# Turning the hidden rows of a routed feed-forward layer through DVE squares and HBM, one expert slot at a time

## What is computed

```python
def _moe2_ref(x, expert_emb, tau, w1, w2):
    ...
    expert_idx = np.argmax(logits, axis=1)
    ...
    for e in range(E):
        mask = expert_idx == e
        ...
        h = np.maximum(x[mask] @ w1[e], 0.0)
        out[mask] = gate_w[mask, None] * (h @ w2[e])
```

## Time and profile before

| | us |
|---|---|
| median of 3 runs (525.84 to 526.74) | 526.49 |
| the profiled execution, its own time | 526.66 |
| its span, first to last instruction | 524.9 |
| TensorE busy in it | 511.5 |
| DVE, ScalarE, GpSimd busy | 332.2, 213.2, 92.5 |

### The profile page before, as it was taken

One profiled execution on the slowest core, in us unless ns is written; L12 is line 12 of the kernel. 1 busy time (PEld: TensorE's weight loads), 2 busy tenths in 40 slices (PEclk: granted clock), 3 DMA queues, 4 the chain that ended last, 5 costly groups with the idle time before them and its releaser, 6 DMA issues.

```text
span 524.9 us, 11573 instructions
## 1 busy us (share of the span) xinstructions
PE 511.5 (97%) x3754; PEld 439.7 (84%) x3755; DVE 332.2 (63%) x712; ACT 213.2 (41%) x480; POOL 92.5 (18%) x223
## 2 busy tenths in 40 slices
PE   8799999999999999999999999999999999999994
PEld 7588888888888888888898999887788888888883
DVE  3679899687867665767554568767573473222662
ACT  5668654433443334333432445441531441111440
POOL 6412121002340000000000001002221211111221
PEclk9999999999999999999999999999999999999999
DMA  8899415586445335332412710102964155101000
GB/s 193 259 340 314 89 35 117 133 150 122 105 117 109 66 66 138 74 61 51 120 42 61 301 41 18 33 33 72 353 225 168 40 183 191 40 29 37 20 20 25
DMA packets 125899, 60.24 MB, mean 115 GB/s; under 512 B 95382, under 2 KB 113814, under 8 KB 125856
## 3 DMA queue, kind: packets, MB, share of 16 engines
q1 hardware_dynamic: 123456, 53.38, 37.4%
q0 software_dynamic: 2400, 6.30, 3.6%
HBM read 50.22 MB, written 11.01 MB: 117 GB/s over the span
## 4 chain that ended last, share of the span: by engine, by line
PE 94%; SPq 2%; DMA 1%; issue 1%; ACT 1%; DVE 0%; POOLq 0%; DVEq 0%; ACTq 0%
PE bank L1051 26%; PE bank L1095 9%; PE bank L1102 9%; PE bank L1108 8%; PE bank L1258 5%; PE bank L1304 5%; PE bank L1266 5%; PE bank L1312 5%; PE bank L1260 5%; PE bank L1306 5%; PE bank L1029 3%; PE bank L1296 2%; PE bank L999 2%; DMA v_raw<-in_v 1%; PE bank L1163 1%
## 5 line engine op out<-in xcount | busy, mean ns | idle before, releaser
L1459 ACT ACTIVATE el<-bank 128x512 f32<-128x512 f32 x48 | 28.6, 597 | 98.4 <-PE bank L1051 98.1
L1051 PE MATMUL bank<-x_hi,w_hi_parts 128*128 128x256 f32 x376 | 60.8, 284 | 0.0
L1051 PE MATMUL bank<-x_lo,w_hi_parts 128*128 128x256 f32 x376 | 60.1, 282 | 0.0
L1051 PE MATMUL bank<-x_hi,w_lo_parts 128*128 128x256 f32 x376 | 60.0, 282 | 0.0
L1051 PEld LDWEIGHTS bank<-x_hi,w_hi_parts 128*128 128x128 f32 x376 | 53.4, 188 | 3.7 <-issue 0.2
L1783 DVE TENSOR_SCALAR el<-el 128x512 f32<-128x512 f32 x48 | 20.6, 429 | 55.0 <-ACT el L1459 55.0
L1095 PE MATMUL bank<-w_hi_parts,g_hi 128*128 128x512 f32 x192 | 54.9, 407 | 0.0
L1102 PE MATMUL bank<-w_lo_parts,g_hi 128*128 128x512 f32 x192 | 52.7, 396 | 0.0
L1108 PE MATMUL bank<-w_hi_parts,g_lo 128*128 128x512 f32 x192 | 52.2, 393 | 0.0
L789 POOL COPY kb<-kT 128x96 f32<-128x96 f32 x96 | 26.2, 316 | 143.7 <-PE bank L999 123.3
L1051 PEld LDWEIGHTS bank<-x_lo,w_hi_parts 128*128 128x128 f32 x376 | 51.3, 188 | 0.0
(11 more groups left out here) (292 smaller groups left out, 871.6 us busy)
## 6 DMA issues: line engine op xcount, KB each, us to landing
raw<-in_moe_w SPq DMA_DIRECT2D x8, 2048.0 KB, 8.9
w_raw<-in_moe_w_in SPq DMA_DIRECT2D x8, 512.0 KB, 6.4
w_raw<-in_moe_w_out SPq DMA_DIRECT2D x8, 512.0 KB, 6.5
p_rows<-p_all SPq DMA_DIRECT2D x16, 256.0 KB, 2.4
p_squares<-p_rows SPq DMA_DIRECT2D x64, 64.0 KB, 2.4
v_raw<-in_v SPq DMA_DIRECT2D x8, 384.0 KB, 4.5
x_rows<-x SPq DMA_DIRECT2D x6, 512.0 KB, 3.2
x<-x_rows SPq DMA_DIRECT2D x20, 128.0 KB, 2.8
```

Of the source, the lines that this page charges most:

```text
L1051: mm = pe.matmul(o, r32(w[:, at:at + P]), r32(x[i % 2][:, c, :]), start=(part == "hh" and c == 0), stop=(part == "lh" and c == DC - 1))
L1459: act.activation(el[n % 2], bank[:, H_BANK[n % 2], :], ACT.Exp).then_inc(e_act, 1)
```

## The change

From slot 2 on `h_sb` is no longer made by ScalarE and transposed by TensorE. DVE transposes the 32x32 squares of the two banks into `h_sb` (`turn_h`, before the ReLU), ScalarE's queue stores `h_sb` to a tensor `h_rows` in HBM (`store_h`) and loads it back in four pieces, each for 32 partitions, into `h_squares` (`load_h`). ScalarE takes the ReLU and the high part from there (`h_high`), DVE the low part in four pieces (`h_low`). A partition then holds other rows of `w2` than before, so `w2` is loaded in four DMAs of 32 partitions (on SyncE's queue), and slots 0 and 1 write `h_sb` in a permuted order.

`down(s)` now follows `up(s + 2)`. Ups of slots 2, 3 and 4 come before the loop, slot 3's in banks 2 and 3 with its own buffers for the turned rows; the last two downs come after the loop. `w1` of a new run is split one pass earlier (in pass s for a start at s+3), and run 1 is entered at slot 4. Slot s's result is stored by DVE behind the `h_low` of slot s+1.

```diff
@@ TensorE
             def up(s):
...
-                pe.wait_ge(h1_ev, s + 1)
+                if isinstance(s, int) and s == FILL:
+                    pe.wait_ge(h1_ev, FILL + 1)
+                elif isinstance(s, int) and s == FILL + 2:
+                    pe.wait_ge(h_turned, 1)
+                elif not isinstance(s, int):
+                    pe.wait_ge(h_turned, s - FILL)
...
+                if isinstance(s, int):
+                    transpose_x(s + 1)
+                up_low(range(HALVES), base, s).then_inc(h1_mm, 1)
...
-            up(2)
-            transpose_x(3)
-            transpose_h(2)
-            up(3)
-            transpose_x(4)
-            down(2)
+            third_last = pe.value_load(tab[0:1, USED, 1:2], min_val=NT - 3, max_val=NSLOT - 3)
+            up(FILL)
+            up(FILL + 1)
+            up(FILL + 2)
+            down(FILL)
             with pe.Fori(FILL + 1, NSLOT) as s:
-                with pe.If(s < used):
-                    transpose_h(s)
-                    with pe.If(s + 1 < used):
-                        transpose_x(s + 2)
-                        up(s + 1)
+                with pe.If(s + 2 < used):
+                    transpose_x(s + 3)
+                    up(s + 2)
                     down(s)
+            down(third_last + 1)
+            down(third_last + 2)
@@ ScalarE
+            def store_h(s):
+                act.wait_ge(h_turned, s - 1)
+                if not isinstance(s, int) or s > FILL:
+                    act.wait_ge(ld_h, 16 * GROUPS * (s - FILL))
+                    carry_waits(act)
+                act.dma_start(h_rows, h_sb).then_inc(st_h, 16)
+            def load_h(s):
+                act.wait_ge(st_h, 16 * (s - 1))
+                if isinstance(s, int) and s == FILL:
+                    act.wait_ge(r_mm, NB)
+                else:
+                    act.wait_ge(hT_ev, 2 * s + 2)
+                    carry_waits(act)
+                for r in range(GROUPS):
+                    act.dma_start(h_squares[r * SQ:(r + 1) * SQ, :].rearrange("p (g d) -> p g d", g=GROUPS),
+                                  h_rows[:, r * FC2 * SQ:(r + 1) * FC2 * SQ].rearrange("(g p) d -> p g d", p=SQ)
+                                  ).then_inc(ld_h, 16)
+            def h_high(s):
+                act.wait_ge(h2_high, s)
+                act.wait_ge(ld_h, 16 * GROUPS * (s - 1))
+                for a in range(2):
+                    act.activation(r32(of_half(hT_hi, a)), h_by_chunk(a), ACT.Relu).then_inc(hT_hi_a, 1)
...
-            relu_halves(FILL)
+            store_h(FILL)
             there, run = starting_run(act, slice(3, 4))
             with act.If(there > 0):
                 high_w1(run())
+            load_h(FILL)
+            there, run = starting_run(act, slice(4, 5))
+            with act.If(there > 0):
+                high_w1(run())
+            store_h(FILL + 1)
...
             with act.Fori(FILL, NSLOT) as s:
...
+                with act.If(s + 2 < used):
+                    h_high(s)
+                    load_h(s + 1)
+                    high_of_next(s)
+                    there, run = starting_run(act, s + 3)
                     with act.If(there > 0):
                         high_w1(run())
...
+                    store_h(s + 2)
+            h_high(third_last + 1)
+            load_h(third_last + 2)
+            high_of_next(third_last + 1)
+            h_high(third_last + 2)
@@ VectorE
+            def turn_h(s):
+                dve.wait_ge(h1_mm, s + 1)
...
+                    dve.wait_ge(st_h, 16 * (s - FILL))
+                b = banks_of_hidden(s)[0]
+                dve.transpose(h_sb, bank[:, b:b + 2, :].rearrange("p a n -> p (a n)")).then_inc(h_turned, 1)
+            def h_low(s):
+                dve.wait_ge(h2_mm, s + 1)
+                dve.wait_ge(hT_hi_a, 2 * s + 2)
+                for r in range(GROUPS):
...
+                    ins = dve.scalar_tensor_tensor(out=r32(lo), in0=rows, scalar=0.0, in1=hi,
+                                                   op0=ALU.max, op1=ALU.subtract)
+                ins.then_inc(hT_ev, 2)
...
-            store_xsT(3)
             store_y(1, list_gate[:, 0, 1:2])
+            dve.wait_ge(meta_v, 2)
+            store_xsT(FILL + 1)
+            turn_h(FILL)
...
+            store_xsT(FILL + 2)
+            there, run = starting_run(dve, slice(4, 5))
+            with dve.If(there > 0):
+                low_w1(run())
+            turn_h(FILL + 1)
...
+            h_low(FILL)
+            turn_h(FILL + 2)
+            store_xsT(FILL + 3)
             later_splits(FILL)
...
             with dve.Fori(FILL + 1, NSLOT) as s:
...
+                with dve.If(s + 2 < used):
+                    h_low(s)
+                    gated_y(s - 1)
                     later_splits(s)
...
+                    turn_h(s + 2)
+                    store_xsT(s + 3)
+            h_low(third_last + 1)
+            gated_y(third_last)
+            low_of_next(third_last + 1)
+            h_low(third_last + 2)
+            gated_y(third_last + 1)
+            gated_y(third_last + 2)
```

More of the change, by code:

```diff
@@ L325, in build @@
          _, _, emb, emb_n,
-         h_sb, hT_hi, hT_lo, slot_vals, _, xs_even) = zone(
+         h_sb, hT_hi, hT_lo, slot_vals, _, xs_even, _, h_squares) = zone(
             "x",
@@ L410, in starting_run, with banks_of_hidden, homes_of_turned_rows, h_by_chunk @@
             return load(0), lambda: load(1)
+        xsT_of_three = tuple(c_free[:, a * DM:(a + 1) * DM].rearrange("p (c n) -> p c n", c=DC) for a in range(2))
+        def banks_of_hidden(s):
+            return HT if isinstance(s, int) and s == FILL + 1 else H1
+        def homes_of_turned_rows(s):
+            return xsT_of_three if isinstance(s, int) and s == FILL + 1 else (xsT_hi, xsT_lo)
+        def h_by_chunk(a):
+            return h_squares.rearrange("p (r c t) -> p c r t", r=GROUPS, c=FC2)[:, 4 * a:4 * a + 4, :, :]
+        def of_half(x, a):
+            return x[:, 4 * a:4 * a + 4, :].rearrange("p c (r t) -> p c r t", r=GROUPS)
         def bank_of_rows(s):
@@ L1305, in down_high @@
                           start=(f == 0), stop=False)
-                pe.matmul(bank[:, 4, :], r32(hT_hi[:, f, :]), r32(W_LO[:, bass.ds(at, DM)]),
-                          start=False, stop=False)
+                return pe.matmul(bank[:, 4, :], r32(hT_hi[:, f, :]), r32(W_LO[:, bass.ds(at, DM)]),
+                                 start=False, stop=False)
             def down_low(s, a, base):
@@ L1589, in relu, with relu_half @@
                 act.wait_ge(h1_mm, s + 1)
[L1590 to L1593, removed]
+                act.wait_ge(h1_t, 2 * s)
+                relu_half(0)
+                relu_half(1).then_inc(h1_ev, 1)
+            def relu_half(a):
+                rows = h_sb.rearrange("p (c q f) -> p q c f", c=FC2, q=GROUPS)[:, 2 * a:2 * a + 2, :, :]
+                return act.activation(rows, bank[:, a, :].rearrange("p (q c f) -> p q c f", q=2, c=FC2), ACT.Relu)
             def hT_high(s):
@@ L1619, in _ @@
             store_x2T(1, S_BANK[1])
[L1620 to L1628, removed]
+            act.wait_ge(h1_half, 1)
+            relu_half(0)
+            act.wait_ge(h1_mm, 1)
+            relu_half(1).then_inc(h1_ev, 1)
             hT_high(0)
@@ L2160, in later_splits @@
                     low_w2(run())
-                there, run = starting_run(dve, s + 2)
+            def later_splits(s):
+                low_of_next(s)
+                there, run = starting_run(dve, s + 3)
                 with dve.If(there > 0):
```

108 lines of the change are left out of this document (57 added, 51 removed).

## The result

The changed kernel takes 571.32 us (median; 569.71 to 573.12) against 526.16 for the kernel before beside it: a ratio of 1.086, interval 1.083 to 1.089. It is 45 us slower. The direction was forecast, the size was not: 543.5 was forecast, and 571.3 lies above the range of 529 to 556. The profiled execution has a span of 568.0, 43.1 over the one before.

The account below looks back on a forecast made before the run. TensorE, 97% busy, was taken as the bound: 526.66 us, less 11.0 for the turns and a wait gone, plus 27.8 of new waits (way in, passes with a split, way out), gives 543.5; range 529 to 556.

Parts of the forecast that it names:

- passes with a split: Row turns wait for xsT behind DVE's and ScalarE's chain: 5.0 in pass 3, 3.2 in 4, 1.6 in 6, 2.4 in 10.
- the way in: Ahead of and entering the loop: the first down waits 5.5 us for slot 2's hidden rows, then down(3) 0.5.
- the way out: Last two downs wait for DVE's stored result: down(12) 5.1 us, skipped passes included, down(13) another 4.5.
- The three durations taken for the turn and the two parts: On DVE and ScalarE: turn_h 1.4 us, h_low 1.6, h_high 2 x 0.6.
- the price of the trip: Hidden rows through HBM: a 512 KB store lands after 3.2 us, a 128 KB load after 2.8.
- the clock: Rival, 15%: TensorE's clock falls in three gaps of 5 us or more, costing 8.4 us; time 552.
- w2 in four DMAs: On SyncE's queue: three more issues, about 1.4 us, with nothing queued behind them for a whole pass; no cost.
- a pass without a split: In the loop: DVE's and ScalarE's work fits, so a pass takes 11.6 us, nothing beyond the matmuls.
- The second up covers it: Rival, 12%: with brief issues on ScalarE, split passes nearly close; way in and passes lose under 3 us; time 524.4.
- Rows come late in every pass: Rival, 8%: GpSimd's gather behind the scatter takes 12.3 us, not 10.9 of 11.6; nine passes lose 0.7 each; 550.

Follow-up runs that it names:

- run 1: Not a follow-up run: within the kernel, the slots from slot 4 on that share one set of new weights w1 and w2; no measured time of its own.
- small weights: The changed kernel, loading only a sixteenth of every row of the new weights (outputs of their slots wrong): 553.2 us, ratio 1.052 to the kernel before.
- order and small weights together: The best order without holding back run 1's w2, and only a sixteenth of every row of the new weights loaded (outputs wrong): 523.8 us, ratio 0.997.
- the best order: The changed kernel with run 1's w2 load held back, casts before load_h, last two passes inside the loop, result stored before h_low: 538.9 us, ratio 1.026.

## Why the prediction was wrong

**Direction and mechanism held.** The chain through DVE and ScalarE in passes with a split, the way in, and the way out were all found where the steps put them: five waits for xsT behind passes 3, 4, 6, 10 (and a short one ahead of pass 3), one for `hT_hi`, two for `y_sb`. The three durations taken for the turn and the two parts were 4 to 12% high.

**The step that failed is the price of the trip.** "Going through HBM is shown for x_rows: a store of 512 KB lands after 3.2, a load of 128 KB after 2.8" was taken for every pass, with crowding granted in the way in alone, and there by 0.7 us in the sum. But new weights are loaded as soon as a split has freed their place, and the next trip starts behind the same split. So the trip behind each of the first splits is crowded, and it hurts where the next pass has a split too: stores took 9.8, 8.0 and 9.0 for slots 2, 3 and 5. Against the steps: first down 11.5 for 5.5; ahead of pass 3 1.7, where the steps had 0.5 at down(3); pass 3 3.3 for 5.0; pass 4 6.7 for 3.2; pass 6 2.5 for 1.6 and pass 10 2.9 for 2.4, both with an uncrowded trip; way out 7.8 for 9.6. With small weights these waits are 19.6 and the time 18 us less, where the steps without their crowding had 27.1. That is the control: the places were right, the price of the trip was too low, and what passes 3 and 4 lose without crowding had been put too high (2.1 for 8.7), which hid a part of the miss.

**The second is the clock.** By the table it is the larger part of the miss. The forecast had +16.8 and the span +43.1. Of these 26.3 us, 8.5 are the waits that the steps name (36.3 for 27.8), 3.5 those for "issue" less the rest of the waits before, and 14.3 the slow matmuls and what was not taken apart. In the run with small weights the slow matmuls come to 12.7, and it ends 10 us above the forecast though the loads crowd nothing. The clock stood among the rivals at 8.4 us for three gaps. It is not a rival but a part of the forecast: slow matmuls stood behind eight of the waits, the ones of 1.66 to 11.5 us, 10.1 us of slower matmuls. In the trace before it was only seen to fall late in an idle of 6 us, and so I counted only gaps of 5 us and more, and gave the whole a chance of 15%. The price on the path is smaller than the sum (nothing at the first gap, about 1.4 us in the way out). The Trainium skill (TensorE: Matmul & The Clock Gate, HAM oscillation) describes bursts that start cold behind a long wait for DMA; the windows of 0.53 and 1.00 above agree.

**Third, two terms at nothing.** w2 in four DMAs was costed at 1.4 us of SyncE's time with nothing behind it; alone, with the permuted rows, it costs 5 us on the kernel before, where ScalarE is behind its landing. And a pass without a split was put at 11.6; with short waits for "issue" ahead of its up (0.53 in pass 9), whose cause was not looked for, passes 8 and 9 took 11.8 and 12.5. Such waits are 4.0 us in all, 1.2 of it ahead of the loop.

**The rivals.** "The second up covers it" fell: four issues hold ScalarE's queue 1.8 us, as SyncE's were held. The rule on issuing engines (the Trainium skill, DMA: Bandwidth & Descriptors, Issuing engines are not separate DMA queues) calls that small relative to the DMA; here it is 1.8 beside a landing of 2.9, and the traces disagree with "small". The same section says that DMAs of all issuing engines run on the same 16 DMA engines and interleave; the stores of ScalarE's queue that took 8.0 to 9.8 us beside a load of SyncE's agree with that half. "Rows come late in every pass" fell: no wait for a gather in the changed kernel.

## What to carry to other kernels

A round trip through HBM must be priced with the transfers that are in flight at that moment, not with the median of a quiet stretch; look up when the big loads are issued, and expect even a transfer of few bytes to be late beside them, as the 64 KB here. On an engine that casts and also issues DMAs, put what another engine waits for next ahead of a DMA whose semaphore is late: here that order alone was worth 16 us. And when work leaves a TensorE that was hardly ever idle, a new gap can cost twice, once as a wait and once as a slow burst behind it, where nothing else sets the pace (some 1.4 us in the way out here, nothing at the first gap).

## What the runs showed of the hardware

- Beside a 2 MB load, a store of 512 KB landed after 8.0 to 9.8 us (five stores of the changed kernel) and one of 64 KB in four pieces a row after 7.0 and 10.9; with the weight loads cut to a sixteenth, 512 KB landed after 2.9.
- TensorE's clock: slow matmuls stood behind a wait of 1.66 us in a stretch with other gaps, down(2) having begun slow itself; in the run of order and small weights together, whose longest wait was 1.5 us, there was none, nor behind a wait of 1.62 in the best order.
- A DVE transpose of 32x32 squares over 1024 columns, PSUM to SBUF, takes 1.25 us, less than twice the 0.694 of 512 columns in SBUF.
- On the kernel before, 2 MB in four DMAs of 32 partitions each were complete 19.5 us after the first issue beside another 2 MB load, where a single DMA took 14.1.
